# Attention, MLP and mixture of experts in one kernel: when the first MLP weights are loaded, how GpSimd's split is cut, which path stands first, and where TensorE issues the first MLP block

## What is computed

```
scores = q @ k.T / sqrt(64)                  # per head, 768 x 768
keep   = key < n_sink or 0 <= query - key < window      # n_sink 4, window 128
x      = softmax(where(keep, scores, -1e9)) @ v          # heads side by side: 1536 x 512
x      = relu(x @ w_in)**2 @ w_out                       # w_in 512 x 2048, w_out 2048 x 512
logits = x @ w_gate + log1p(exp(x @ w_noise)) * noise    # 8 experts
out    = sum over the best two e: weight * relu(x @ w1[e]) @ w2[e]   # F = 1024
```

## Time and profile before

| | |
|---|---|
| median of 3 runs | 782.74 us |
| the profiled execution | 783.07 us, of which 781.3 us span |
| mean granted clock of PE | 0.976 of full |
| busy: PE, DVE, ACT, POOL | 94%, 41%, 36%, 14% of the span |
| attention | up to about 118.7 us |
| MLP, router, experts | from there to 781.3 us |

### The profile page before, as it was taken

How to read it: one execution, slowest core, us unless ns; L and a number is a source line. 1 busy time by engine, 2 the same in 40 slices (tenths; PEclk the granted TensorE clock), 3 DMA queues, 4 the chain that set the end, 5 groups by cost and what they waited for, 6 DMA issues and landing times.

```text
span 781.3 us, 12123 instructions
## 1 busy us (share of the span) xinstructions
PE 731.9 (94%) x4844; PEld 619.1 (79%) x4844; DVE 321.1 (41%) x728; ACT 279.3 (36%) x533; POOL 112.6 (14%) x99
## 2 busy tenths in 40 slices
PE   5588998999999999999998999999999999999992
PEld 4477876888778888888887889898988888898981
DVE  5487872542221532225654173524343433425200
ACT  4455762431232322223432163425242333434210
POOL 5291000000000040000503210201111020202011
PEclk9888998999999999999999999999999999999997
DMA  7954628920000020004434517382817355372122
GB/s 231 333 156 131 213 72 317 372 90 1 0 1 1 2 108 3 0 0 170 155 134 179 151 35 262 41 284 28 268 43 195 124 130 187 60 266 31 24 28 29
DMA packets 40282, 94.80 MB, mean 121 GB/s; under 512 B 6176, under 2 KB 6176, under 8 KB 40224
## 3 DMA queue, kind: packets, MB, share of 16 engines
q1 hardware_dynamic: 33696, 79.17, 29.1%
q0 software_dynamic: 6528, 14.83, 9.6%
HBM read 68.24 MB, written 25.75 MB: 120 GB/s over the span
## 4 chain that ended last, share of the span: by engine, by line
PE 87%; DVE 4%; DMA 3%; ACT 3%; issue 1%; SPq 0%; POOL 0%; DVEq 0%; ACTq 0%; POOLq 0%
PE ps L1384 22%; PE ps L1369 21%; PE ps L1296 17%; PE ps L1286 16%; PE ps L1211 2%; PE ps L1179 2%; PE ps L1357 2%; DMA k_sb<-kT 2%; ACT s_probs L569 1%; PE ps L1192 1%; DVE s_inv L803 1%; PE ps L1193 1%; PE ps L1313 1%; DVE s_probs L790 1%; PE ps L1307 1%
## 5 line engine op out<-in xcount | busy, mean ns | idle before, releaser
L1384 PE MATMUL ps<-w_hi,hT_hi 128*128 128x512 f32 x256 | 102.8, 401 | 0.0
L1384 PE MATMUL ps<-w_hi,hT_lo 128*128 128x512 f32 x256 | 100.4, 392 | 0.0
L1384 PE MATMUL ps<-w_lo,hT_hi 128*128 128x512 f32 x256 | 100.0, 391 | 0.0
L1023 DVE TENSOR_TENSOR w_lo<-w_raw,w_hi 128x2048 fp32r<-128x2048 f32 x36 | 82.6, 2294 | 37.0 <-ACT w_hi L648 37.0
L526 POOL DMA_INDIRECT out<-y_sb,meta_tok x32 | 50.5, 1578 | 286.5 <-DVE meta_w L1066 139.4
L1074 DVE SCALAR_TENSOR_TENSOR hT_lo<-ps,hT_hi 128x448 fp32r<-128x448 f32 (+2 forms) x64 | 39.8, 624 | 122.9 <-ACT hT_hi L686 122.8
L907 DVE SCALAR_TENSOR_TENSOR g_sb<-ps,g_sb 128x512 f32<-128x512 f32 x48 | 33.2, 692 | 120.1 <-ACT g_sb L614 118.9
L614 ACT ACTIVATE g_sb<-ps 128x512 f32<-128x512 f32 x48 | 28.7, 598 | 143.3 <-PE ps L1286 143.3
L686 ACT ACTIVATE hT_hi<-ps 128x448 fp32r<-128x448 f32 (+2 forms) x64 | 34.7, 544 | 123.8 <-PE ps L1369 123.8
L1296 PE MATMUL ps<-w_hi,gT_hi 128*128 128x512 f32 x192 | 76.6, 399 | 0.5 <-DVE gT_lo L909 0.3
L515 POOL DMA_INDIRECT expert_rows<-x_rows,slots_i x24 | 26.8, 1117 | 344.4 <-DVE slots_i L1013 338.0
(11 more groups left out here) (161 smaller groups left out, 1168.2 us busy)
## 6 DMA issues: line engine op xcount, KB each, us to landing
w_raw<-w SPq DMA_DIRECT2D x32, 1024.0 KB, 9.2
xg<-expert_rows SPq DMA_DIRECT2D x32, 262.0 KB, 11.1
v_sb<-v SPq DMA_DIRECT2D x8, 832.0 KB, 4.6
expert_rows<-pad_rows SPq DMA_DIRECT2D x24, 262.0 KB, 3.8
w_raw<-w_in SPq DMA_DIRECT2D x4, 1024.0 KB, 8.5
w_raw<-w_out SPq DMA_DIRECT2D x4, 1024.0 KB, 12.7
vt_sb<-v_tail SPq DMA_DIRECT2D x8, 480.0 KB, 7.1
k_sb<-kT SPq DMA_DIRECT2D x8, 456.0 KB, 8.0
```

The source lines that it names most:

```text
L1023: dve.tensor_tensor(piece(w_lo, s, i), piece(w_raw, s, i), piece(w_hi, s, i).bitcast(F32), ALU.subtract).then_inc(ready, 1)
L1384: m = pe.matmul(ps[:, Y_BANKS[t % 2], :], a[:, f, rows_of(t)], w[:, slot, l2_cols(f)], start=(f == 0 and k == 0), stop=(f == HALF_F - 1 an ...
```

## The change

Five edits:

- SP: the first half's weight loads leave the place before the attention block. In the windowed path pieces 0 and 1 are issued behind the v loads of pair 2, pieces 2 and 3 behind those of pair 3. Each piece has a semaphore of its own.
- POOL: the split waits for one piece at a time and runs in pieces of 512 columns: 16 casts and 16 subtractions in place of 4 and 4.
- ACT, DVE, PE, SP: the general block stands before the windowed one, so its jump lies before attention.
- PE: the 12 matmuls of `layer1(0, 0)` are issued between `s_output(23)` and `s_turn(22)`. They wait for the split and for the first 12 batches' `x_lo_done`.
- PE: the waits for `attn_done` and the router tensors move behind MLP group 0.

```diff
-            for i in range(4):
-                sp.dma_start(piece(w_raw, 0, i), mlp_source(0, i)).then_inc(mlp_w_in, 16)
+            def load_first(i):
+                sp.dma_start(piece(w_raw, 0, i), mlp_source(0, i)).then_inc(mlp_w_in[i], 16)
...
                     sp.wait_ge(s_pv, PB * (pair - 1))
                     load_v(pair, pair % 2)
+                    if pair < 4:
+                        load_first(2 * pair - 4)
+                        load_first(2 * pair - 3)
...
-                pool.tensor_copy(piece(w_hi, s, i), piece(w_raw, s, i)).then_inc(pool_steps, 1)
+                cols = slice(i * PIECE + k * QUARTER, i * PIECE + (k + 1) * QUARTER)
+                pool.tensor_copy(w_hi[:, 0, cols], w_raw[:, 0, cols]).then_inc(pool_steps, 1)
...
-            pool.wait_ge(mlp_w_in, 16 * 4)
             for i in range(4):
-                split(0, i, mlp_w_split)
+                pool.wait_ge(mlp_w_in[i], 16)
+                for k in range(4):
+                    split(i, k)
...
+              pe.wait_ge(attn_done, 1)
+              layer1(0, 0, True)
+            with pe.If(short == 1):
...
                     s_output(n)
+                    if n == BATCHES - 1:
+                        pe.wait_ge(x_lo_done, PB * DC)
+                        layer1(0, 0, True)
                     if n >= 1:
                         s_turn(n - 1)
                 s_turn(BATCHES - 1)
...
-            pe.wait_ge(attn_done, 1)
...
+            mlp_group(0, True)
+            pe.wait_ge(attn_done, 1)
             pe.wait_ge(router_in, 48)
-            mlp_group(0, True)
```

More of the change, by code:

```diff
@@ L221, in build @@
         pool_steps, out_zeroed = sem("pool_steps"), sem("out_zeroed")
-        mlp_w_in, mlp_w_split = sem("mlp_w_in"), sem("mlp_w_split")
+        mlp_w_in, mlp_w_split = [sem(f"mlp_w_in{i}") for i in range(4)], sem("mlp_w_split")
         scores_done, scores_masked, probs_done, inv_done = sem("scores_done"), sem("scores_masked"), sem("probs_done"), sem("inv_done")
@@ L345, in _ @@
                              a.rearrange("(c p) e -> p c e", p=P)).then_inc(router_in, 16)
-            for i in range(4):
-                sp.dma_start(piece(w_raw, 0, i), mlp_source(0, i)).then_inc(mlp_w_in, 16)
+            def load_first(i):
+                sp.dma_start(piece(w_raw, 0, i), mlp_source(0, i)).then_inc(mlp_w_in[i], 16)
             sp.wait_ge(short_ready, 1)
             short = sp.value_load(is_short[:, :], min_val=0, max_val=1)
+            with sp.If(short == 0):
+              for i in range(4):
+                  load_first(i)
+              with sp.Fori(1, PAIRS) as pair:
+                sp.wait_ge(pv_done, 2 * QT * pair)
+                for t, a, landed in ((q_sb[:, 0, :], qT, qk_in), (k_sb[:, 0, :], kT, qk_in),
+                                     (v_sb[:, 0, :, :, :].rearrange("p t h d -> p (t h d)"), v, v_in)):
+                    sp.dma_start(t, a[:, bass.ds(pair, 1), :].rearrange("p a s -> p (a s)")).then_inc(landed[0], 16)
             with sp.If(short == 1):
@@ L496, in _, with split @@
             n_split = [0]
-            def split(s, i, ready):
-                pool.tensor_copy(piece(w_hi, s, i), piece(w_raw, s, i)).then_inc(pool_steps, 1)
+            QUARTER = PIECE // 4
+            def split(i, k):
+                cols = slice(i * PIECE + k * QUARTER, i * PIECE + (k + 1) * QUARTER)
+                pool.tensor_copy(w_hi[:, 0, cols], w_raw[:, 0, cols]).then_inc(pool_steps, 1)
                 n_split[0] += 1
                 pool.wait_ge(pool_steps, 7 + n_split[0])
-                pool.tensor_tensor(piece(w_lo, s, i), piece(w_raw, s, i), piece(w_hi, s, i).bitcast(F32),
-                                   ALU.subtract).then_inc(ready, 1)
-            pool.wait_ge(mlp_w_in, 16 * 4)
+                pool.tensor_tensor(w_lo[:, 0, cols], w_raw[:, 0, cols], w_hi[:, 0, cols].bitcast(F32),
+                                   ALU.subtract).then_inc(mlp_w_split, 1)
             for i in range(4):
-                split(0, i, mlp_w_split)
+                pool.wait_ge(mlp_w_in[i], 16)
+                for k in range(4):
+                    split(i, k)
             def scatter(g):
@@ L583, in _ @@
             short = act.value_load(is_short[:, :], min_val=0, max_val=1)
+            with act.If(short == 0):
+              with act.Fori(0, BATCH) as b:
+                with act.Fori(0, DC) as c:
+                    for qt in range(QT):
+                        for hh in range(2):
+                            soften((b * DC + c) * (2 * QT) + 2 * qt + hh)
+                        act.wait_ge(oT_done, (b * DC + c) * QT + qt + 1)
+                        act.activation(xT_hi[:, bass.ds(c, 1), bass.ds(b * SEQ + qt * P, P)].rearrange("p a s -> p (a s)"),
+                                       ps[:, 5, 0:P], ACT.Copy).then_inc(x_hi_done, 1)
             with act.If(short == 1):
@@ L595, in _ @@
                 s_high(BATCHES - 1)
[L596 to L604, removed]
             def mlp_step(g, f, first):
@@ L820, in _ @@
             short = dve.value_load(is_short[:, :], min_val=0, max_val=1)
[L821 to L837, removed]
             a_step, bias_steps = sem("a_step"), sem("bias_steps")
@@ L896, in _ @@
               dve.sem_inc(attn_done, 1)
+            with dve.If(short == 1):
+                s_mask(0)
+                s_mask(1)
+                s_copy_tail(0)
+                s_invert(0)
+                for n in range(BATCHES):
+                    if n + 2 < BATCHES:
+                        s_mask(n + 2)
+                    if n + 1 < BATCHES:
+                        s_copy_tail(n + 1)
+                        s_invert(n + 1)
+                    s_norm(n)
+                    if n >= 1:
+                        s_low(n - 1)
+                s_low(BATCHES - 1)
+                dve.wait_ge(x_lo_done, BATCHES)
+                dve.sem_inc(attn_done, 1)
             dve.wait_ge(consts_done, 1)
@@ L1225, in s_turn, with layer1 @@
                 t.then_inc(s_oT, 1)
+            def layer1(g, f, first):
+                b = f % 2
+                s, fl = f // HALF_F, f % HALF_F
+                n = FC1 * g + f
+                if first and fl == 0:
+                    pe.wait_ge(mlp_w_split, 16 + 4 * s)
+                if not (first and f < 2):
+                    pe.wait_ge(m_sq, n - 1)
+                for i, (w, x) in enumerate(((w_hi, xT_hi), (w_hi, xT_lo), (w_lo, xT_hi))):
+                    for c in range(DC):
+                        m = pe.matmul(ps[:, 4 + b, :], w[:, s, l1_cols(c, fl * P, P)], x[:, c, bass.ds(g * GROUP, GROUP)],
+                                      start=(i == 0 and c == 0), stop=(i == 2 and c == DC - 1))
+                m.then_inc(m_l1, 1)
             pe.wait_ge(short_ready, 1)
             short = pe.value_load(is_short[:, :], min_val=0, max_val=1)
[L1229 to L1242, removed]
             with pe.If(short == 0):
@@ L1269, in _ @@
                     pe.wait_ge(x_lo_done, pair * QT + qt + 1)
-            pe.wait_ge(attn_done, 1)
[L1274 to L1288, removed]
+              pe.wait_ge(attn_done, 1)
+              layer1(0, 0, True)
+            with pe.If(short == 1):
+                s_score(0)
+                s_score(1)
+                pe.wait_ge(consts_done, 1)
+                s_transpose(0)
+                for n in range(BATCHES):
+                    if n + 2 < BATCHES:
+                        s_score(n + 2)
+                    if n + 1 < BATCHES:
+                        s_transpose(n + 1)
+                    s_output(n)
+                    if n == BATCHES - 1:
+                        pe.wait_ge(x_lo_done, PB * DC)
+                        layer1(0, 0, True)
+                    if n >= 1:
+                        s_turn(n - 1)
+                s_turn(BATCHES - 1)
             def layer2(g, f):
@@ L1325, in mlp_group @@
                 for f in range(FC1):
-                    layer1(g, f, first)
+                    if not (first and f == 0):
+                        layer1(g, f, first)
                     if f >= 1:
```

## The result

The changed kernel takes 777.12 us (median of 9 runs, 774.52 to 778.93) against 782.74 for the kernel before (9 runs, 780.81 to 785.39): a ratio of 0.9924 [0.9909, 0.994]. It is faster by 5.6 us where 17.6 were forecast, and lies outside the range. The profiled execution took 776.28 us, its span 774.4, 6.9 less than before; the mean granted clock of PE is 0.981.

A forecast was written before the change was run, and what follows sets the result against it. PE, busy 94%, was taken to bound the kernel, its gaps lying in the first 130 us. From 783.07, -19.0 + 0.6 + 0.6 + 4.1 - 3.9 gave 765.5, or 765.1 us as median; range 759 to 773.

The forecast's parts named there:

- the three causes: Attention, batches 6 to 12: late pair 2 k 8.40, half clock after it 2.75, adds held beside POOL's split 7.84 us.
- The jump in front, +4.1: Start of attention: general block first makes DVE pay its jump before its first mask, +4.1 us.
- The bound of 6: Upper bound in us on the jump at the start, given because the DMA engines are loaded then.
- PE has cover: Start: PE's jump is covered, since its first scores start at 8.20 and DVE's first mask comes only at 11.57.
- Queue of pairs 3 and 4 and POOL, +1.2: Attention: +0.6 us for q and k of pairs 3 and 4 behind weights, +0.6 for adds still waiting on POOL.
- rival B: Weights keep their toll: pairs 3 and 4 each 4.8 us late plus clock, +14.6, 779.7 us; chance 0.15.
- just meets: The argument for B, on the load queue of pairs 3 and 4: demand just meets supply.
- POOL's residual, +0.6: Some 8 batches beside the split: randomly arriving adds exceed DVE's slack by 0.07 us each in the mean, +0.6 us.
- The end, -3.9: End of attention: early layer1(0, 0) brings layer 2 to 9.34 us after s_output(23) from 13.23, gain 3.89 us.
- what would make it wrong: Signs of failure, among them half clock through the first MLP blocks, which would take 2.6 us of the gain.
- C, a free jump: Start: the jump's target is already at hand and costs nothing, 761.0 us; chance 0.20.
- D, DVE held through a chain of pieces: Beside the split: adds wait for a chain of two POOL pieces, 12.8 us, +27.3, 792.4 us; chance 0.03.

The follow-up runs named there:

- q and k only: Changed kernel with SP issuing only q and k of pair 0 before s_score(0) is done, all other loads after: 776.79 us, 0.9921.
- early weights: Changed kernel with the first half's weight loads back at their old place ahead of attention, behind the router tensors: 777.04 us, 0.9917.
- spread weights: Changed kernel with the four weight pieces issued one a pair, behind q and k of pairs 3 to 6: 775.6 us, 0.9885.

## Why the prediction missed

**Where attention lost time: right.** Batch 6 has no idle before it, no add is over 1.28 us, and the 19.0 us of the three causes are gone. What came in their place is what was mis-sized.

**The jump in front, +4.1: the term of the sum that was mis-sized, 8.3 measured.** The price came from a stretch where little was being loaded, to be paid where two pairs were in flight. The bound of 6 named that and stopped short. Its "PE has cover" held for the 3.4 us before the first mask, not for a 7.45 us gap and another of 2.26 us inside its first scores. With idle DMA engines PE's first score comes 4.68 us behind k (q and k only); under loads it is 6.0 to 7.5 for PE, and 5.8 us for DVE, each its own.

The Trainium skill (Runtime: NRT & Kernel Launch, Instruction fetch mechanics) says that a branch outside the pages held fetches by DMA. The traces agree: the first score comes at 12.20, 13.88 and 15.22 us as the load grows, each time 2.7 to 3.2 us behind a packet of 16 KB on the instruction queue. The same section calls the cost of crossing into the next block "mostly hidden". That is so for most packets, but the 2.26 us, and the 1.42 and 1.65 us above in straight code, are the same wait, each 2.6 to 3.3 us behind a packet.

**Queue of pairs 3 and 4 and POOL, +1.2: mis-sized, 5.8 measured.** It was rival B's mechanism at some 40% of its price of 14.6, within the bound. From the issue of v to the landing of k the sum had 11.2 + 2.4 = 13.6 us for both pairs. For pair 3 it took 49.18 - 33.61 = 15.6; for pair 4 48.52 - 44.04 = 4.5 us passed before SP had issued k (q's issue alone took 2.51), and k landed 13.93 us after that: 18.4. The chain of waits has this last step as one piece:

```profile
48.52 13.93 DMA k_sb<-kT
```

A queue that "just meets" demand has no slack for either. The clock behind batch 12 (1.6) is in the 5.8 too. The gap of 0.80 us at 60.10 is not: k came at 62.45, and PE would only have waited longer for it. But the toll could not be had back: early weights gave 0, spread weights 1.5 us at most, and gaps by "issue" stood elsewhere in both.

**POOL's residual, +0.6: wrong in kind, small here.** The sum took random arrivals. The adds arrive in step, 0.34 us a batch (3.82 - 3.48) instead of 0.07. It shows in the kernel with pieces alone, 1.1 us in its trace; in the changed kernel adds of 1.18 and 1.26 us stand in batches 3.48 apart, and the third, of 1.25 us, stands ahead of the wait on k of batch 12.

**The end, -3.9: the number right, 9.31 for 9.34, the reason wrong.** The whole step was credited to the early layer 1. With the early block and the jump at the end it is 13.04 us, 0.2 less than before; with the jump in front and no early block 8.72 (all else as changed) and 10.33 (general block first alone, where layer1(0, 0) ran at half clock in part). So the gain is the jump's move, and that the sum came out is luck. With it in front, layer 1 starts right after attn_done and still hides the table load. What the early block adds is an idle stretch of 1.83 us before layer 2, and in the changed kernel half the clock behind it, 1.6 us. The prediction named that among what would make it wrong, at 2.6 us, and gave it no chance. That the idle brings the clock down is not shown: 1.83 us and 1.76 us of idle stand before a layer 2 at full clock in two other traces, and the half clock of the 10.33 came without such a stretch. The comparison missing on paper was the changed kernel with this edit left out.

**Rivals.** B came in part (above). C, a free jump, and D, DVE held through a chain of pieces, did not come. With pieces of 512 columns no add took over 1.28 us.

**Left open.** Why a code packet comes too late at some places and not at others, and why these move with each kernel; whether DVE's 5.8 us are the same wait (its own code packets were not followed); and what decides the clock behind layer 2's idle. Late weights and early layer 1 were not run alone on the kernel before.

## What to carry to other kernels

Price a jump, or anything else that may need the DMA engines, by the load in flight where it is put, and for each engine by itself. Here the cheap place was the end of attention, where the loads were done and the stalls of PE and DVE lay side by side. Look at the instruction queues in the profile's view of the DMA engines when a gap has no other cause. Cost every edit of a bundle also against the bundle without it: late weights and early layer 1 were each priced against the kernel before, and were worth nothing or less once the jump had moved. When one engine's instruction holds another's in a loop, reckon with their falling in step, and cut the pieces below the slack rather than near it.

## What the runs showed of the hardware

- The same jump over a block cost 3.0 us of PE at the end of attention; at the start PE's first score came 4.7 us behind k with idle DMA engines, 6.0 behind one pair's loads, 7.5 behind two; of DVE it cost 3.8 to 5.8 us.
- PE's code comes in packets of 16 KB on a DMA queue of its own, and each of the 45 gaps by "issue" of 0.4 us or more ended 2.4 to 3.7 us after one.
- Straight code has gaps by "issue" of 0.5 to 3 us, at different places in each kernel.
- The add of 128 x 4 on DVE takes as long as the rest of POOL's subtraction, 1.25 to 1.27 us for 512 columns where it meets all of it, and the loop can lock to POOL's cycle (3.82 us a batch, 2 x 1.91). POOL's own instructions take 0.61 and 1.28 us for 512 columns against 1.88 and 4.54 for 2048.
- A relu inside attention needed no table load, and the 1.28 us load came all the same ahead of the first relu behind the blocks.
- After an idle of 1.83 us, 12 matmuls ran 4.61 us instead of 3.05 in the changed kernel; after 1.83 us in another kernel and 1.76 us in a third they ran at full clock.
